# Softmax exponential taken from the score banks, with the negated row maximum as bias and the row sum as second output

## What is computed

```python
# q, k, v: (8, 8, 576, 64); chunks of 64 positions; scale = 1/8
scores = scale * q_c @ k_c^T                     # 64 x 64 for each chunk and head
scores = scores - max(scores, axis=-1)
attn = exp(scores)
attn = attn / (sum(attn, axis=-1) + 1e-9)
out = attn @ v_c
x = out as (4608 tokens, 512)
h = x @ w_in;  x = (max(h, 0) + alpha * min(h, 0)) @ w_out      # 512 -> 2048 -> 512
h = x @ w2_in; x = (h - tanh(h)) @ w2_out
```

## Time and profile before

| | |
|---|---|
| median of three executions | 1587.15 us (1586.89 to 1588.39) |
| the profiled execution's own time | 1585.87 us |
| its span | 1584.1 us |
| PE busy | 1561.9 us (99%) |
| DVE busy | 979.0 us (62%) |
| ACT busy | 619.2 us (39%) |
| POOL busy | 314.6 us (20%) |

### The profile page before, as it was taken

One profiled execution on the slowest core, in us unless ns is written; L12 is line 12 of the kernel. 1 busy time (PEld: TensorE's weight loads), 2 busy tenths in 40 slices (PEclk: granted clock), 3 DMA queues, 4 the chain that ended last, 5 costly groups with the idle time before them and its releaser, 6 DMA issues.

```text
span 1584.1 us, 26708 instructions
## 1 busy us (share of the span) xinstructions
PE 1561.9 (99%) x10512; PEld 1480.5 (93%) x10512; DVE 979.0 (62%) x1371; ACT 619.2 (39%) x947; POOL 314.6 (20%) x434
## 2 busy tenths in 40 slices
PE   6999999999999999999999999999999999999999
PEld 5999999999999999999999989989989988988987
DVE  7987677668768766775864644653653652662642
ACT  5566335535534543553542322332331331241231
POOL 4974440051034015004564200000000000000000
PEclk8999999999999999999999999999999999999999
DMA  7695994697578579549879837636735735844741
GB/s 253 246 338 180 368 321 171 211 336 263 178 279 286 184 245 332 214 140 358 283 248 339 294 133 271 234 133 245 265 144 212 296 141 188 302 151 160 280 182 67
DMA packets 83146, 375.04 MB, mean 237 GB/s; under 512 B 10064, under 2 KB 23376, under 8 KB 48464
## 3 DMA queue, kind: packets, MB, share of 16 engines
q1 hardware_dynamic: 73136, 341.35, 59.8%
q0 software_dynamic: 9600, 31.46, 5.4%
q10 hardware_dynamic: 288, 0.52, 0.1%
HBM read 308.29 MB, written 65.01 MB: 236 GB/s over the span
## 4 chain that ended last, share of the span: by engine, by line
PE 93%; DVE 3%; issue 1%; DMA 1%; POOL 1%; ACT 0%; SPq 0%; DVEq 0%; ACTq 0%
PE banks L597 14%; PE banks L599 14%; PE banks L598 14%; PE banks L626 8%; PE banks L628 8%; PE banks L627 8%; PE banks L660 6%; PE banks L661 6%; PE banks L659 5%; PE a_bank L660 3%; PE a_bank L659 3%; PE a_bank L661 3%; POOL ring L409 1%; PE a_bank L535 1%; DMA ring<-w_split 1%
## 5 line engine op out<-in xcount | busy, mean ns | idle before, releaser
L597 PE MATMUL banks<-xo_hi,ring 128*128 128x384 f32 x1344 | 450.9, 336 | 2.7 <-DMA ring<-w_split 1.5
L599 PE MATMUL banks<-xo_hi,ring 128*128 128x384 f32 x1344 | 450.2, 335 | 0.0
L598 PE MATMUL banks<-xo_lo,ring 128*128 128x384 f32 x1344 | 450.1, 335 | 0.0
L1107 DVE TENSOR_TENSOR go_lo<-g_full,go_hi 128x768 fp32r<-128x768 f32 x288 | 281.2, 982 | 231.6 <-ACT go_hi L847 230.8
L847 ACT CAST go_hi<-g_full 128x768 fp32r<-128x768 f32 x288 | 239.8, 837 | 362.0 <-PE banks L661 223.8
L626 PE MATMUL banks<-go_hi,ring 128*128 128x384 f32 x768 | 260.4, 339 | 1.5 <-DVE go_lo L1107 1.1
L597 PEld LDWEIGHTS banks<-xo_hi,ring 128*128 128x128 f32 x1344 | 253.1, 188 | 5.2 <-issue 2.8
L628 PE MATMUL banks<-go_hi,ring 128*128 128x384 f32 x768 | 256.8, 334 | 0.0
L627 PE MATMUL banks<-go_lo,ring 128*128 128x384 f32 x768 | 256.7, 334 | 0.0
L598 PEld LDWEIGHTS banks<-xo_lo,ring 128*128 128x128 f32 x1344 | 253.1, 188 | 0.4
L599 PEld LDWEIGHTS banks<-xo_hi,ring 128*128 128x128 f32 x1344 | 253.0, 188 | 0.0
(11 more groups left out here) (130 smaller groups left out, 1839.9 us busy)
## 6 DMA issues: line engine op xcount, KB each, us to landing
ring<-w_split SPq DMA_DIRECT2D x242, 1024.0 KB, 6.4
w_split<-ring SPq DMA_DIRECT2D x22, 1024.0 KB, 5.1
qkv<-in_chunks SPq DMA_DIRECT2D x60, 256.0 KB, 5.3
w_split<-made_first POOLq DMA_DIRECT2D x44, 256.0 KB, 6.8
w_split<-sums POOLq DMA_DIRECT2D x44, 256.0 KB, 6.8
y_between<-stage SPq DMA_DIRECT2D x12, 768.0 KB, 8.0
x_raw<-y_between SPq DMA_DIRECT2D x6, 1536.0 KB, 10.7
out<-x_raw SPq DMA_DIRECT2D x36, 256.0 KB, 6.5
```

Of the source, the lines that this page charges most:

```text
L597: nc.tensor.matmul(h, hi, xo_hi[:, o, k, :], start=fresh and k == 0, stop=False, skip_group_check=not fresh)
L598: nc.tensor.matmul(h, hi, xo_lo[:, o, k, :], start=False, stop=False, skip_group_check=not fresh)
L599: last = nc.tensor.matmul(h, lo, xo_hi[:, o, k, :], start=False, stop=k == 1, skip_group_check=not fresh)
L1107: nc.vector.tensor_tensor(go_lo[:, slot, :, :], g_of(n), go_hi[:, slot, :, :], ALU.subtract).then_inc(glo_ready, 1)
```

## The change

The subtraction of the maximum and the row-sum reduction leave DVE. DVE takes the maximum, multiplies its eight values per row by -scale (128 x 8), and stops there. ACT then runs eight exponentials of 128 x 64 for a unit (one for each block and head), straight from the score banks, with a column of the negated maximum as bias and a column of `row_sum` as accumulated second output. `row_max` and `row_sum` get two slots each, by the unit's parity, and the waits follow. In phase B both units of a pair have their `shift` at age 0, and their exponents are moved one unit later on ACT, to ages 1 and 2; `normalize` stays at ages 2 and 3.

```diff
-        row_max, row_sum = sb("row_max", [P, 2, G * UNIT]), sb("row_sum", [P, G * UNIT * 2])
+        row_max, row_sum = sb("row_max", [P, 2, 2, G * UNIT]), sb("row_sum", [P, 2, G * UNIT * 2])
...
             def exponent(u):
-                act.wait_ge(shifted, u + 1)
-                nc.scalar.activation(probs_of(u), probs_of(u), ACT.Exp, scale=scale).then_inc(exp_done, 1)
+                act.wait_ge(shifted, together(u))
+                if u > 1:
+                    act.wait_ge(attn_ready, u - 1)
+                if probs_users(u) > 0:
+                    act.wait_ge(attnT_done, probs_users(u))
+                heads = score_bank(u)
+                for b in range(G * UNIT):
+                    for r in range(2):
+                        last = nc.scalar.activation(probs_of(u)[:, b, r, :], heads[:, r, b * CHUNK:(b + 1) * CHUNK], ACT.Exp,
+                                                    bias=row_max[:, u % 2, r, b:b + 1], scale=scale,
+                                                    accum_out=row_sum[:, u % 2, 2 * b + r:2 * b + r + 1])
+                last.then_inc(exp_done, 1)
...
-                    if age == u % 2:
+                    if age == u % 2 + 1:
                         exponent(UPS * (s + 1) + u)
...
-                if u:
-                    dve.wait_ge(shifted, u)
+                if u > 1:
+                    dve.wait_ge(exp_done, u - 1)
...
-                nc.vector.tensor_reduce(row_max[:, :, :], heads, AXIS_X, ALU.max).then_inc(max_ready, 1)
+                nc.vector.tensor_reduce(row_max[:, u % 2, :, :], heads, AXIS_X, ALU.max).then_inc(max_ready, 1)
                 dve.wait_ge(max_ready, u + 1)
-                if probs_users(u) > 0:
-                    dve.wait_ge(attnT_done, probs_users(u))
-                nc.vector.tensor_tensor(probs_of(u).rearrange("x b r j -> x r b j"), heads,
-                                        row_max[:, :, :].unsqueeze(3).to_broadcast([P, 2, G * UNIT, CHUNK]),
-                                        ALU.subtract).then_inc(shifted, 1)
+                nc.vector.tensor_scalar(row_max[:, u % 2, :, :], row_max[:, u % 2, :, :], -scale, None, ALU.mult).then_inc(shifted, 1)
...
-                nc.vector.tensor_reduce(row_sum[:, :], mine, AXIS_X, ALU.add).then_inc(norm_step, 1)
-                dve.wait_ge(norm_step, 3 * u + 1)
-                nc.vector.tensor_scalar(row_sum[:, :], row_sum[:, :], 1e-9, None, ALU.add).then_inc(norm_step, 1)
+                nc.vector.tensor_scalar(row_sum[:, u % 2, :], row_sum[:, u % 2, :], 1e-9, None, ALU.add).then_inc(norm_step, 1)
...
-                    if age == u % 2:
+                    if age == 0:
                         shift(UPS * (s + 1) + u)
```

More of the change, by code:

```diff
@@ L992, in normalize @@
                     dve.wait_ge(attn_ready, u)
-                nc.vector.tensor_reduce(row_sum[:, :], mine, AXIS_X, ALU.add).then_inc(norm_step, 1)
-                dve.wait_ge(norm_step, 3 * u + 1)
-                nc.vector.tensor_scalar(row_sum[:, :], row_sum[:, :], 1e-9, None, ALU.add).then_inc(norm_step, 1)
-                dve.wait_ge(norm_step, 3 * u + 2)
-                nc.vector.reciprocal(row_inv[:, :], row_sum[:, :]).then_inc(norm_step, 1)
-                dve.wait_ge(norm_step, 3 * u + 3)
+                nc.vector.tensor_scalar(row_sum[:, u % 2, :], row_sum[:, u % 2, :], 1e-9, None, ALU.add).then_inc(norm_step, 1)
+                dve.wait_ge(norm_step, 2 * u + 1)
+                nc.vector.reciprocal(row_inv[:, :], row_sum[:, u % 2, :]).then_inc(norm_step, 1)
+                dve.wait_ge(norm_step, 2 * u + 2)
                 nc.vector.tensor_tensor(mine, mine, row_inv[:, :].unsqueeze(2).to_broadcast([P, G * UNIT * 2, CHUNK]),
```

## The result

The changed kernel takes 1603.91 us (median of four executions, 1601.77 to 1605.18) against 1587.26 us for the kernel before in the same runs: 16.7 us more, a ratio of 1.0102 (95% interval 1.0085 to 1.0120). 1611 had been forecast, in a range from 1589 to 1634. The profiled execution took 1604.09 us, its span 1602.3.

A forecast was written before the change was run, and what follows sets the result against it. PE was taken to bound the kernel, so only its standing still counts. Opening 5.2, phase B 14.4 in runs 1 to 4 and 5.5 in run 0 sum to 25.1 us on 1585.87: 1611 us, range 1589 to 1634.

The forecast's parts named there:

- the two places: The opening, forecast to lose 5.2 us, and phase B, forecast to lose 14.4 us in runs 1 to 4 and 5.5 in run 0.
- the sum of 25.1 us: Whole kernel: 5.2 us in the opening, 14.4 in phase B of runs 1 to 4 and 5.5 in run 0.
- What bounds the kernel: PE, busy 99%: only its standing still counts, and a later end of the opening moves the rest one for one.
- E: Time of one unit's exponent on ACT: 2.8 us claimed, between bounds of 1.4 and 3.7 us.
- my own case: One unit's exponent on ACT takes 2.4 us (1599 us in total) to 3.1 us (1621 us); chance 0.60.
- Opening: Before PE's first product: ACT becomes the chain and ends at 37.2 instead of 32.0 us, a loss of 5.2 us.
- 4E - 6.0: Formula for the opening's loss in us, from the time E of one unit's exponent; 5.2 us at E = 2.8.
- the list: ACT's steps in the opening, start to start, from exponent 2 at 13.84 us to the last copy at 25.99 + 4E.
- Phase B: PE's waits in the pairs: +1.96, +0.4 and +1.25 us in each of runs 1 to 4; +2.6, 1.0 and 1.85 in run 0.
- rival 3: PE's clock falls in its new pauses: 13 us more if once in each first pair, 1624 us; every pair 1650; chance 0.04.
- a sign of being wrong: PE starting later than 40 us with E below 3, or PE losing time where ACT was not late.

The follow-up runs named there:

- experiment 5: The change with the opening's softmax as in the kernel before, phase B as in the change: 1599.76 us, ratio 1.0079 to the kernel before.
- experiment 6: The kernel before with the changed softmax in the opening only, phase B as before: 1592.04 us, ratio 1.0029 to the kernel before.
- Experiment 8: The kernel before with the new softmax only in units 0 and 1 of the opening: 1586.61 us, ratio 1.0002 to the kernel before.
- experiment 4: The change without the exponentials' second output, VectorE summing the rows again: 1595.75 us, ratio 1.0053 to the kernel before.
- experiment 10: The change without the bias column in the eight exponentials, so the row maximum isn't subtracted: 1587.77 us, one execution.
- Experiment 9: The change with act_rest moved from phase-B unit 3 to 4 and activate from unit 5 to 6: 1592.79 us, ratio 1.0031 to the kernel before.
- experiment 2: The change with the old softmax in the opening and, by a slip, phase B's shift and exponent at the old ages 0 and 1: 1633.91 us.
- experiment 11: The change measured once more, unaltered: 1602.69 us, ratio 1.0091 to the kernel before.
- experiment 7: The change with each phase-B unit's eight exponentials cut in two halves behind successive units' high_g: 1609.12 us, ratio 1.0136 to the kernel before.
- experiment 12: The change with act_rest and activate moved behind the first pair, and only units 0 and 1 of the opening changed: 1589.01 us, ratio 1.0005 to the kernel before.
- experiment 3: The change's softmax in the opening; in phase B the old softmax, by a slip at the new ages: 1596.47 us, ratio 1.0055 to the kernel before.

## Why the prediction was right

The direction, the two places and their mechanism held; the sum of 25.1 us was too large, 16.7 was measured.

- **What bounds the kernel.** Right: what the opening loses reaches the end unchanged (experiments 5 and 6), and DVE's relief of 40 us brought no gain over the kernel before. Experiment 8 shows a limit of it: a gain in the opening is stopped by VectorE's `low_x` and the first load of run 1. The prediction also says that what DVE sheds in phase B is worth nothing there. That doesn't hold for the row sum, which in the new order stands between the last exponential and the transposes: with the same E, the kernel that keeps it takes 8 us more (experiments 4 and 10).
- **E.** The mis-sized term. I had put a second instruction's fixed 0.20 us behind each exponential, counted in full, for E = 2.8. It is there, but overlaps its neighbours and costs 0.09 us (experiment 4). The exponential costs 0.20, not 0.15: without a column it takes 0.11, less than I had, and the column, which I had left out, adds 0.09 (experiment 10). E is 2.33 from start to start, just below my own case, which began at 2.4; read as the prediction asked, from the first start to the last end (13.90 to 16.39 us), it is 2.49. From the Trainium skill's figures (ScalarE: Activation LUTs, What ACT_TABLE_LOAD costs) an exponential with a column is estimated at 280 + 53 - 93 = 240 ns, 40 ns above the 0.20 us of this trace.
- **Opening.** 4E - 6.0 gives 3.3 us with E = 2.33; the first product was 4.3 us late, and the parts apart give 5.3. The chain is the one of the list, with two gaps that it lacks: unit 3's exponent waited 0.5 us for the maximum of VectorE, and `copy_x` 2 almost 1 us for PE, whose clock fell to half 3.7 us sooner than before (at 23.31, not 27.02 us).
- **Phase B.** With E = 2.33 the sums of the prediction give +1.0, nothing and +0.3 us for the three pairs of runs 1 to 4, and +2.6 us in run 0 (1.7, 0.1 and 0.9). Measured, matmul by matmul: 1.3, nothing and 0.4, and 3.4 in run 0 (2.8, 0.3 and 0.4; ahead of them 0.6 us come back, where the kernel before has a pause at 100.08 us that the change hasn't). The sum for the first pair of run 0 was too small for a reason on VectorE: the two of `activate` took 2.82 us from start to start, not 2.34, and `low_g(7)` 1.48 us, not 0.95, with POOL at work on low parts beside them. Experiment 9 moved what the list had ahead of `normalize` and `low_g(7)`, and the waits went. The timeline of VectorE in the change, run 0, ahead of unit 7 at 119.59 us:

```profile
115.14 2.90 DVE L1102 SCALAR_TENSOR_TENSOR g_full<-stage,alpha_rest,g_full 128x768 f32<-128x768 f32 x2
117.96 2.88 DVE L1111 TENSOR_TENSOR go_lo<-g_full,go_hi 128x768 fp32r<-128x768 f32 x2
```

- **Not in the sum.** The half clock after the transfer's wait (1.6 us) was rival 3 at a place that it didn't name, and at about a tenth of its price. The pause at 303 us (1.8) was in no case. Together they are 3.4 of the 18.2 us of the profile, and they are what the prediction had named as a sign of being wrong, time that PE loses where ACT was not late. With the right E my sum would have been 11 us, 5 below the measured one; that 25.1 wasn't further off is in part luck, since too long an E stood in for what the sum lacked.

## What to carry to other kernels

An accumulated second output and a column as bias each cost 0.09 us from start to start here: eight small instructions with both take 3.7 times as long as the one that they replace (2.33 against 0.63 us). Moving work between two engines that are both half idle gained nothing here; list what stands ahead of the last deadline on each in-order engine, and move the work that has no deadline there (here `act_rest` and `activate`, 10 to 11 us) before moving the work that has. Exponents one unit earlier cost 9 us, and 34 us where the second maximum came a unit later as well, so an order must be worked out for both deadlines: of the work moved and of what now stands behind it.

## What was not expected of the hardware

- The clock of PE after a pause. A pause of 3.3 us went with 3.4 or 6.8 us at 0.50 each time (the third pairs of runs 0 to 4 in experiment 2). Of pauses with 1.9 to 2.2 us of idle time and dense work before and after, some were followed by it (1.99 us at 182.59 in the change, 2.15 in experiment 11, 1.90 at 115.82 in experiment 5, 2.13 at the transposes of run 0 in experiment 7) and some weren't (1.87 at 119.59 in the change, 1.96 at the same transfer in experiment 9, 2.19 at 175.08 in experiment 8). What decides between them stays open.
- A pause of PE in the middle of a unit, waiting for no other engine, in run 1 of the change (1.68 us), of experiments 11 (1.41) and 12 (1.68), shorter in experiment 5 (0.58) and hardly there in experiment 3 (0.15), each time at the same matmul of PE's program; in the kernel before and in experiment 9 it is absent. The records of single packets in the traces show what goes with it. Queue q8, of the kind "instruction", moves 86 packets of 16 KB in each of the fourteen profiles, and PE's program is the same in all of them, while queue q14 of the same kind goes from 36 to 39 packets as ScalarE's program grows; so q8 is taken here to bring PE's instructions. In all fourteen profiles PE stands still for more than 0.1 us without a named wait 16 times after the first products, at four places of its program, and each time it goes on 2.2 to 2.6 us after the start of the latest packet of q8. In the change that packet starts at 300.83 us, in the kernel before 4.9 us ahead of the same matmul, in experiment 9 2.9 us. Before and inside the pause of the change (columns as in the earlier trace rows, then the queue's packets, MB and share of 16 engines from 300.80 to 303.11 us):

```profile
294.70:300.80 6.10, 6.10 (x94) 5.78 (x93) 5.22 (x6) 4.24 (x7) 0.00 (x0) 1.00 0.86 289
300.80:303.11 2.31, 0.63 (x5) 0.48 (x4) 0.00 (x0) 0.01 (x1) 0.00 (x0) 1.00 0.04 10
```

```profile
q8 instruction: 1, 0.02, 2.6%
```

  So the pauses fit a block of PE's instructions that comes late. What makes it start late isn't shown, and no experiment moved it on purpose.
- Durations of ScalarE's rows swell along a run without gaps (an exponential from 0.30 to 0.42 us) while the starts keep their step of 0.29 us.
